# Convolution tiles of 128 rows, seven to a group, with the six halo rows as a matmul of their own

## The reference

```python
# 1: causal convolution, 7 taps, 8 heads of 24 channels, taps = softmax of weight
x_pad = np.concatenate([np.zeros((B, pad, D)), x], axis=1)
out = np.einsum('hk,bskhg->bshg', w, x_unf)
# 2: mixture of 8 experts, only where x @ w_skip > 0; the rest keeps x
y = gate_w * (np.maximum(xc @ w1[e], 0.0) @ w2[e]);  out = xc + y
# 3: a second mixture of 8 experts on every token, logits + modality_bias[modality_id]
out = gate_w * (np.maximum(x @ w1[e], 0.0) @ w2[e])
```

## Time and profile before

| | us |
|---|---|
| median of 3 runs (lowest, highest) | 1223.38 (1221.72, 1226.15) |
| the profiled execution | 1223.26 |
| its span, first to last instruction | 1221.6 |
| share of the span in which the PE was busy | 92% |
| mean granted clock of the PE | 0.942 |

### The profile page before, as it was taken

The page is one execution under the profiler, slowest core; times in us unless marked ns, Lnnn a source line. Parts: engine busy times, 40 slices in busy tenths (PEclk is TensorE's granted clock), DMA queues, the critical chain, the costliest instruction groups (busy, mean ns, idle before and its releaser), DMA issues.

```text
span 1221.6 us, 27087 instructions
## 1 busy us (share of the span) xinstructions
PE 1121.5 (92%) x8431; PEld 1081.7 (89%) x8432; DVE 661.2 (54%) x1942; ACT 457.6 (37%) x867; POOL 462.2 (38%) x582
## 2 busy tenths in 40 slices
PE   5888989719999999999959999999999999999996
PEld 5777777609999999999949999999999999999996
DVE  4545555556867777777855444444444444444444
ACT  2423333214545535544515333333333333333333
POOL 5345555553433244424424322222333322333224
PEclk9878878858999999999989999999999999999998
DMA  5644444135333243243225111111111111111110
GB/s 153 177 122 124 127 126 121 51 109 141 112 100 102 65 116 111 60 120 114 59 89 161 40 40 42 45 40 40 40 40 43 40 43 40 40 40 40 41 45 22
DMA packets 85357, 97.13 MB, mean 80 GB/s; under 512 B 26706, under 2 KB 76198, under 8 KB 85330
## 3 DMA queue, kind: packets, MB, share of 16 engines
q1 hardware_dynamic: 68138, 66.26, 20.3%
q0 software_dynamic: 15072, 28.47, 7.3%
q10 hardware_dynamic: 2120, 2.09, 0.5%
HBM read 65.01 MB, written 33.54 MB: 81 GB/s over the span
## 4 chain that ended last, share of the span: by engine, by line
PE 82%; issue 8%; DVE 3%; another core or an unknown queue 3%; ACT 1%; SPq 1%; DMA 1%; POOL 0%; ACTq 0%; DVEq 0%; POOLq 0%
PE banks L1033 36%; PE banks L1046 22%; PE banks L1042 10%; PE banks L503 2%; DVE valid L1161 1%; PE banks L501 1%; PE banks L1025 1%; PE banks L1022 1%; PE banks L1023 1%; PE banks L218 1%; PE banks L515 1%; PE banks L516 1%; PE banks L528 1%; PE banks L219 1%
## 5 line engine op out<-in xcount | busy, mean ns | idle before, releaser
L1033 PE MATMUL banks<-xt,w_up 128*128 128x256 f32 x3600 | 450.6, 284 | 2.6 <-ACT xt L1106 2.3
L1033 PEld LDWEIGHTS banks<-xt,w_up 128*128 128x128 f32 x3600 | 447.2, 190 | 3.7 <-ACT xt L1106 2.6
L1046 PE MATMUL banks<-w_dn,hid_hi 128*128 128x384 f32 (+1 forms) x1440 | 434.7, 365 | 0.0
L1125 ACT ACTIVATE hid_hi<-banks 128x512 fp32r<-128x512 f32 x360 | 213.9, 597 | 502.8 <-PE banks L1033 468.3
L1042 PE MATMUL banks<-w_dn,hid_lo 128*128 128x192 f32 (+1 forms) x1440 | 356.4, 255 | 0.0
L1219 DVE SCALAR_TENSOR_TENSOR hid_lo<-banks,hid_hi 128x512 fp32r<-128x512 f32 x360 | 245.1, 690 | 193.8 <-ACT hid_hi L1125 160.5
L1042 PEld LDWEIGHTS banks<-w_dn,hid_lo 128*128 128x128 f32 x1440 | 273.8, 191 | 0.0
L1046 PEld LDWEIGHTS banks<-w_dn,hid_hi 128*128 128x128 f32 x1440 | 270.4, 188 | 0.0
L328 POOL DMA_INDIRECT out<-y_both,idx x114 | 112.1, 983 | 247.6 <-DVE y_both L1212 217.2
L975 POOL TENSOR_TENSOR split<-ahead,split 128x256 fp32r<-128x256 f32 x94 | 65.3, 695 | 285.7 <-ACT split L1110 285.5
L480 POOL DMA_INDIRECT buckets<-rows,idx x128 | 121.3, 947 | 120.0 <-DVE idx L799 70.7
(11 more groups left out here) (198 smaller groups left out, 1208.7 us busy)
## 6 DMA issues: line engine op xcount, KB each, us to landing
ahead<-buckets SPq DMA_DIRECT2D x94, 202.0 KB
x_in<-in_x SPq DMA_DIRECT2D x16, 672.0 KB
stage<-in_w SPq DMA_DIRECT2D x11, 768.0 KB
kept<-buckets SPq DMA_DIRECT2D x33, 202.0 KB
stage<-in_w SPq DMA_DIRECT2D x11, 512.0 KB
stage<-in_w SPq DMA_DIRECT2D x22, 256.0 KB
w_turned<-in_w_t SPq DMA_DIRECT2D x8, 512.0 KB
w_turned<-in_w_t SPq DMA_DIRECT2D x8, 256.0 KB
```

Source lines behind the costliest of these rows:

```text
L1033: mm = nc.tensor.matmul(o, w_up[:, slot, w, f * P:(f + 1) * P], xt[:, a * UNIT:(a + 1) * UNIT], start=(m == 0), stop=(m == len(terms) - 1))
L1046: mm = nc.tensor.matmul(p_y[:, t, 0:2 * COLS], hid_hi[:, f, c], w_dn[:, slot, f, :, 0:COLS], start=(f == 0), stop=(f == FT - 1))
L1125: nc.scalar.activation(hid_hi[:, 2 * b:2 * b + 2, :], p_h[:, b % HB, :].rearrange("p (f c) -> p f c", f=2), ACT.Relu).then_inc(hi_done, 1)
```

## The change

A tile has 128 rows instead of 112 and a group 7 tiles instead of 8, so a group still has 896 tokens and there are still 16 groups. As 128 rows fill the partitions, the six halo rows get a buffer `x_halo` of their own (on partitions 0 to 5 for even groups and 32 to 37 for odd ones), and the part of the band that multiplies them gets its own tile, which shares the memory of `line`, with one copy for each place. Each head then takes two matmuls of 168 columns into the same PSUM region, one over 128 rows and one over 6; in the first group of a sequence the second has 144 columns. The halves of transposes, splits and logits have 4 and 3 tiles instead of 4 and 4. `bias1` moves into the memory of `rows`, slot 3.

```diff
-    TP, TG = 112, 8
+    TP, TG = 128, 7
+    H0 = (TG + 1) // 2
-    KP = TP + HALO
-    LINE = KP + TP
+    LINE = HALO + 2 * TP
...
-        line = sb("line", [1, HEADS, LINE])
-        band = sb("band", [KP, HEADS, TP])
+        halo_parts = 32 + HALO
+        line_store = sb("line", [halo_parts, HEADS * LINE])
+        line = line_store[0:1, :].rearrange("p (h c) -> p h c", c=LINE)
+        band_halo = line_store[:, 0:HEADS * TP].rearrange("p (h m) -> p h m", m=TP)
+        band = sb("band", [TP, HEADS, TP])
+        x_halo = sb("x_halo", [halo_parts, TG, D])
...
-        bias1 = sb("bias1", [TP, NT, E])
+        bias1 = rows[:, 3, :, :].rearrange("p t c -> p (t c)")[:, 0:NT * E].rearrange("p (t j) -> p t j", j=E)
...
+            halo_of = lambda k: slice(k % 2 * 32, k % 2 * 32 + HALO)
+            TILES = (range(0, H0), range(H0, TG))
+            ROWS = tuple(slice(r[0] * TP, (r[-1] + 1) * TP) for r in TILES)
...
-                        sp.dma_start(x_in[TP:KP, k % 2, :, :], src.rearrange("(t p) d -> p t d", p=TP)[0:HALO])\
+                        sp.dma_start(x_halo[halo_of(k), :, :], src.rearrange("(t p) d -> p t d", p=TP)[0:HALO])\
...
-                sp.wait_ge(band_loaded, 32)
+                sp.wait_ge(band_loaded, 48)
...
-                        if k == 0:
-                            nc.tensor.matmul(o[:, 0, :], band[0:TP, head, :], x_in[0:TP, k % 2, 0, cols], start=True, stop=True)
-                            mm = nc.tensor.matmul(o[:, 1:TG, :], band[:, head, :], x_in[0:KP, k % 2, 1:TG, cols], start=True, stop=True)
-                        else:
-                            mm = nc.tensor.matmul(o, band[:, head, :], x_in[0:KP, k % 2, :, cols], start=True, stop=True)
+                        t0 = 1 if k == 0 else 0
+                        nc.tensor.matmul(o, band[:, head, :], x_in[:, k % 2, :, cols], start=True, stop=False)
+                        mm = nc.tensor.matmul(o[:, t0:TG, :], band_halo[halo_of(k), head, :], x_halo[halo_of(k), t0:TG, cols], start=False, stop=True)
...
-                    for t in range(TG // 2):
+                    for t in TILES[half]:
...
-                    for at in range(TG // 2):
+                    for at, t in enumerate(TILES[half]):
...
-                act.dma_start(band[0:TP, :, :], bass.AP(taps_line, 0, [[1, TP], [LINE, HEADS], [1, TP]])).then_inc(band_loaded, 16)
-                act.dma_start(band[TP:KP, :, :], bass.AP(taps_line, TP, [[1, HALO], [LINE, HEADS], [1, TP]])).then_inc(band_loaded, 16)
+                act.dma_start(band[:, :, :], bass.AP(taps_line, 0, [[1, TP], [LINE, HEADS], [1, TP]])).then_inc(band_loaded, 16)
+                for k in range(2):
+                    act.dma_start(band_halo[halo_of(k), :, :], bass.AP(taps_line, TP, [[1, HALO], [LINE, HEADS], [1, TP]])).then_inc(band_loaded, 16)
```

More of the change, by code:

```diff
@@ L31, in conv_two_moes @@
     NT = N // TP
-    assert NT == P and GB == 4 and NG == 16
-    KP = TP + HALO
+    assert NT <= P and TP == P and GB == 4 and NG == 16
     CL = 2 * E
@@ L511, in transpose @@
                         pe.wait_ge(logits_read, i * 2 + (half - 1))
-                    for t in range(TG // 2):
-                        o = slice(t * TP, (t + 1) * TP)
-                        row = rows[:, k, half * (TG // 2) + t, :]
+                    for t in TILES[half]:
+                        o = slice((t - TILES[half][0]) * TP, (t - TILES[half][0] + 1) * TP)
+                        row = rows[:, k, t, :]
                         nc.tensor.matmul(p_xt8[:, half, 0, o], row[:, 0:DA], ident[0:TP, 0:TP], start=True, stop=True, is_transpose=True)
@@ L521, in logits @@
                     pe.wait_ge(xt_read, i * 2 + (half + 1))
-                    for at in range(TG // 2):
+                    for at, t in enumerate(TILES[half]):
                         o = p_log[:, half, at, :]
-                        t = half * (TG // 2) + at
                         c = slice(t * TP, (t + 1) * TP)
@@ L544, in tensor @@
                 pe.wait_ge(consts, N_CONSTS)
-                nc.tensor.matmul(p_rank[0:TP, 0:NT], mod_f[:, :], ident[:, :], start=True, stop=True, is_transpose=True).then_inc(mod_t_done, 1)
+                nc.tensor.matmul(p_rank[0:TP, 0:NT], mod_f[:, :], ident[0:NT, 0:NT], start=True, stop=True, is_transpose=True).then_inc(mod_t_done, 1)
                 pe.wait_ge(mod_t_read, 1)
@@ L550, in tensor @@
                     nc.tensor.matmul(p_fold[:, 0:P], ident[:, :], ident[:, :], start=True, stop=True)
-                pe.wait_ge(band_loaded, 32)
+                pe.wait_ge(band_loaded, 48)
                 def first_ranked(i, b, k):
@@ L626, in hi_xt @@
                     act.wait_ge(xt_ready, i * 2 + (half + 1))
-                    at = half * (TG // 2) * TP
-                    nc.scalar.activation(xt8[:, 0:3:2, at:at + (TG // 2) * TP], p_xt8[:, half, :, 0:(TG // 2) * TP], ACT.Copy)\
+                    n = len(TILES[half]) * TP
+                    nc.scalar.activation(xt8[:, 0:3:2, ROWS[half]], p_xt8[:, half, :, 0:n], ACT.Copy)\
                       .then_inc(xt_hi, 1)
@@ L746, in lo_xt @@
                     dve.wait_ge(xt_hi, i * 2 + (half + 1))
-                    at = slice(half * (TG // 2) * TP, (half + 1) * (TG // 2) * TP)
-                    n = (TG // 2) * TP
+                    at = ROWS[half]
+                    n = len(TILES[half]) * TP
                     hi = xt8.bitcast(F32)
@@ L758, in read_logits @@
                     dve.wait_ge(logits_done, i * 2 + (half + 1))
-                    part = lg[:, half * (TG // 2):(half + 1) * (TG // 2), :]
-                    link(nc.vector.tensor_copy(part, p_log[:, half, :, NLE:NLE + NL]))
-                    nc.vector.tensor_tensor(part, part, p_log[:, half, :, 0:NL], ALU.add).then_inc(logits_read, 1)
+                    n = len(TILES[half])
+                    part = lg[:, TILES[half][0]:TILES[half][0] + n, :]
+                    link(nc.vector.tensor_copy(part, p_log[:, half, 0:n, NLE:NLE + NL]))
+                    nc.vector.tensor_tensor(part, part, p_log[:, half, 0:n, 0:NL], ALU.add).then_inc(logits_read, 1)
                 def route(i, b, k):
```

4 lines of the change are left out of this document (2 added, 2 removed).

## The result

The changed kernel takes 1339.15 us (median of 4 runs, 1331.28 to 1369.12) against 1222.55 us for the kernel before (1219.82 to 1226.15): a ratio of 1.093, 95% interval 1.0852 to 1.1009. I had forecast 1216 us, with 1207 to 1229 as the range. Six executions of the changed kernel fall into two clusters, three at 1331 to 1344 us and three at 1363 to 1369 us with a lower mean clock; the ratio is that of the first three. The direction was wrong and the size is outside everything I had priced.

The account below looks back on a forecast made before the run. POOL's burst of scatters, not the PE, was taken to set the regular step (14.27 us). Steps -5.7, end of stage -3.0, start +1.0, with 0.4 given back, took 1223.26 to 1216.0 us; range 1207 to 1229.

Parts of the forecast that it names:

- The pair of heads on the PE: Convolution matmuls: priced by columns, a pair goes from 0.66 to 1.16 us, mean 1.72 us more per step.
- The clock: PE in regular steps: 2.8 us a step lost to the lower clock, expected to shrink, perhaps to 1.4, with idle time.
- Rival B: Convolution steps: PE takes over at the lower clock, every second step 16.8 us, 1230 us in all; chance 0.16.
- The scatters: POOL's bursts: 7 scatters instead of 8 per group, slots of 1.29 instead of 1.257 us, loop 1.02 us shorter.
- rival C: POOL's bursts: release waits for 896 rows written, however many scatters, so neither loop nor end shortens; 1229 us; chance 0.09.
- The loop of 13.25 us: Regular steps: release, seven scatters, next release take 13.25 us instead of 14.27; with late PE steps, mean 14.1.
- The start and the mixtures: Before the regular steps about +1 us, 0.3 of it from the band; mixtures' 953 us unchanged, above 2 us wrong.
- The rule that I set beside my bound: Halo matmul on the PE: by the skill's rule, 32 rows take the time of 128, so the pair costs the upper value.

Follow-up runs that it names:

- after_again: The changed kernel, unchanged, run and traced on another chip, where the kernel before takes 1224.4 us: 1339.6 us.
- shift: Changed kernel without halo buffer; the second matmul reads all 128 rows of the tile before, against a band zero but for six rows: 1198.9 us, ratio 0.9835.
- halo_z64: Changed kernel with 64 zero rows ahead of the six in the halo matmul, 70 rows in all: 1202.5 us, ratio 0.984.
- before_again: The kernel before, unchanged, run again for a trace on a chip like the first: 1225.5 us.
- halo_z96_b: Changed kernel with 96 zero rows ahead of the six in the halo matmul, 102 rows, run a second time: 1197.9 us, ratio 0.9835.
- snake: Changed kernel with the second head of a pair turned round (tile, halo, halo, tile), in groups with a tile before them: 1267.8 us, ratio 1.033.

## Why the prediction was wrong, point by point

- **The pair of heads on the PE: the step that failed.** "What a matmul over 6 rows costs no row shows... from above it costs by its columns as all others here do. I take the upper value... The pair then takes 1.16 us." It takes 1.92 us at full clock and 3.4 at the lower one. My upper bound was none: it had the columns and left out the weight load. Every conv matmul of the kernel before covers 112 or 118 rows, so no row of that trace could show a load across a change of height. But it did show that columns are not the whole price, in the second pair of the earlier trace rows, which I misread as "one price per column": its 384 columns took 0.93 us when put at full clock, where the first pair's took 0.66. Beside the two rows of that pair, these two belong to it:

```profile
119.82 0.88 PE L501 MATMUL banks<-x_in,band 118*112 118x168 f32 x2
120.49 0.43 PE L500 MATMUL banks<-x_in,band 112*112 112x24 f32 x2
```

  From the matmul of 24 columns to the next it is 0.26 us (119.56 to 119.82), where 24 columns at 3.44 ns would give 0.08. With 128 against 70, 102 or 128 rows the pair costs 1.15 us, my figure. Four pairs with 0.76 us more make 3.0 us of PE work a step, at full clock.
- **The clock: the term that was mis-sized next.** I allowed 1.4 to 2.8 us a step and argued that the clock rises as the idle time shrinks. The PE's idle time did shrink, to nothing, and the clock fell to 0.57. My 11.8 us of work plus 3.0 are 14.8, near the 14.2 of the steps at clock 1.00; the step lasts 23.7; so 8.9 to 9.5 us went to the clock, where I had 1.4 to 2.8. Without it the step would be no longer than the 14.6 of the kernel before. "Busy" in the records was no measure of what the clock answers to: `after_again` is busy in all of a step at 1.00 and in all of one at 0.57. And a row that I had read spoke against my argument: from 171.3 to 187.5 us the kernel before was busy 15.7 of 16.2 us and had 0.58. In `shift`, where matmuls are tall and unbroken, the clock did rise, to 0.94, as I had argued.
- **Rival B** ("the PE takes over at the lower clock", 1230 us, chance 0.16) named what the trace shows, but neither its cause nor its size: 16.8 us in every second step, where it was 23.6 us or more in ten of the eleven steps from 86.03 to 341.88 us. It took its price from the slowest step of the kernel before, where no matmul is short.
- **The scatters: right.** Slots of 1.28 us against 1.29. The last two bursts start at 367.27 and end with a start at 383.97 us, 16.7 us for 13 slots against 16.8. Below, the end of the stage in the changed kernel, POOL's last scatter of a burst and DVE's reading:

```profile
362.35 0.98 POOL L487 DMA_INDIRECT buckets<-rows,idx  x1 [0.30 <-issue]
```

```profile
364.89 0.23 DVE L766 COPY logit<-banks 128x68 f32<-128x68 f32 x1 [2.71 <-remote]
```

  The release comes 2.54 us after the last scatter's start, behind 7 scatters, against 2.79 behind 8, and with the same 896 rows most steps of `halo_z64` are 12.7 to 12.8 us, where those of `before_again` on the same chip are 14.2. So rival C (the hold follows rows) fell: the step follows the number of scatters.
- **The loop of 13.25 us: right in kind, 0.5 too long.** `shift` shows 12.7 to 12.8 us in most steps and 13.5 and 14.8 in single ones, 13.1 in the mean of eight (103.63 to 208.35 us); I had 14.1. Most of the half microsecond is the release: ACT's reading comes 2.2 to 2.4 us after the last scatter's start there, where I had 2.81. The PE was late less often than I thought; its clock had gone up, which is the likely reason. So the gain that I forecast exists and is larger than forecast, 1.6% instead of 0.6% (`shift` and `halo_z96_b` on their chip); the change as written gives it away many times over.
- **The start and the mixtures.** The first convolution starts 0.14 us later (I took 0.3). The mixtures are 2.5 us longer; I had called anything above 2 wrong. It is 2 in 100 of the loss, and no run looks into it.
- **The rule that I set beside my bound.** "TensorE: Matmul & The Clock Gate" of the Trainium skill, section "Why this matters for your kernels", has the single matmul over 32 rows at the time of one over 128. The trace of `snake` agrees for the matmul itself, 1.53 us for a pair with two matmuls over 6 rows, and I let the agreement of rule and bound pass for a check of the bound. Neither that rule nor my bound speaks of the load in between.

## What to carry to other kernels

Before splitting off a short matmul, count the changes of height in the PE's stream: here each cost 0.19 us at full clock and 0.30 at the lower one (0.86 us against 0.56 in the 70-row version), and the kernels that had them ran most of the stage at the lower clock, which cost far more. If rows must be split off, fill the short matmul with zeros (or with neighbouring data against zero weights) until it counts as tall (here 70 rows did and 64 did not), or put the short ones next to each other. And a cost that the kernel before hides everywhere is not bounded by its trace: ask of each new instruction which of the hidden things, here the weight load, stays hidden beside it.

## What the runs showed of the hardware that I had not expected

- A weight load overlaps the matmul ahead of it between 128 rows and 70, 102 or 128, and between 6 and 6; between 128 and 6, 38 or 64 it does not, in either direction: 0.18 us of idle ahead of it at full clock, 0.36 at the lower one. Where between 64 and 70 the border lies, and whether 6 rows beside 38 would be hidden, was not tried.
- With the PE busy in all of a step and the same exposed loads in it, the granted clock was 1.00 in one step and 0.57 in another of the same execution, 14.25 against 23.43 us. The exposed loads at full clock are 0.77 us x 4 pairs x 16 groups = 49 us of PE time, but the steps at full clock were on average no longer than those of the kernel before: the 118 us of the stage came only with the lower clock.
- On one chip, from 60 to 225 us, the clock was 0.55 with halo matmuls of 6 rows and 0.72 with 64; on another it was 0.70 with 6 rows. The lower rate of the shorter matmul holds in all seven executions on the one chip; its size does not carry over.
- Signals of the PE late in a burst of scatters reach the others only 2.2 to 2.9 us after its last scatter's start in most bursts, on the chips where the kernel before takes 1218 to 1225 us. On the 1177-us chip a reading inside a burst came as the PE ended. What holds the signals, and what differs between the chips, stays open.
